# Log sums in quarters of the array, and a scan that delivers scaled states, in a kernel of decayed linear attention and two feed-forward layers

## The chip, the cores and the metric

The kernel runs on 1 core of one Trainium2 chip. The metric is the device time of one execution in microseconds (us). TensorE is PE in the rows (PEld is its weight load), VectorE is DVE, ScalarE is ACT, GpSimd is POOL, SyncE is SP.

## The reference

Three stages follow each other. `B, H, S, D` are 4, 8, 768, 48; the slots are 32 (8 experts of 4), the hidden widths 1024 and 2048.

```python
def _attn_ref(r, k, v, w, u):
    for t in range(S):
        kt, vt, rt, wt = (k[:, :, t], v[:, :, t], r[:, :, t], w[:, :, t])
        cur = np.einsum('bhd,bhe->bhde', u[None] * kt, vt)
        y[:, :, t] = np.einsum('bhd,bhde->bhe', rt, state + cur)
        state = wt[:, :, :, None] * state + np.einsum('bhd,bhe->bhde', kt, vt)

def _moe_ref(x, phi, w1, w2):
    logits = x @ phi
    d = softmax of logits over the tokens
    slot_input = d.T @ x
    slot_out[e] = np.maximum(slot_input[e] @ w1[e], 0.0) @ w2[e]
    c = softmax of logits over the slots
    return c @ slot_out

def _moe2_ref(x, w_in, w_out):
    h = x @ w_in
    g = h * (1.0 / (1.0 + np.exp(-1.702 * h)))
    return g @ w_out
```

All arrays are float32. The two softmax lines are shortened here.

## The kernel before, in words

Each engine has its own program, written out in order, and they meet at semaphores. The attention works on 16 steps, each a pair of heads of one batch (`pair`). A pair's two heads lie at partitions 0 to 47 and 64 to 111 (`HOFF` is 64, `DP` 112). The 768 tokens are 6 chunks (`NC`) of 128 (`P`).

The decays of a chunk are turned into products of powers. ScalarE takes the logarithm of w (`logs`, L473), TensorE adds it up along the tokens by a product with the constant `tri` (`log_sums`, L897), with the middle token of the chunk (`MID`, 64) as origin: column t of `tri` sums the logs from t to the middle with a minus, or from the middle to t with a plus, and column 64 is zero. ScalarE takes exp of both signs (`exps`, L498 and L500) into `pinv` and `pw`, 129 columns a chunk. VectorE multiplies k by `pinv` and r by `pw` (`front`, L701 and L703) and works out `fdec`, the decay from one chunk's middle to the next's (L705).

Inside a pair TensorE goes in this order: transposes of k (L977), in three of four pairs transposes of the batch before's x (L917), transposes of the previous pair's y (L956), the updates of the state by each chunk (L992, into `bank5`, laid out e outside and chunk inside), the scores k times r (L1010), the log sums of the next pair (L897), the states into y (L1033) and the values into y (L1041). Every f32 product shows as two passes in the trace.

Between the updates and the states into y, ScalarE spreads `fdec` over `frep` (`spread_decay`, L515), VectorE runs one scan over all chunks (L712: state = frep * state + update, 240 elements, the zero in the first chunk's column starts each row anew), and ScalarE scales each chunk's state by `fdec` in five copies into `sc` (`scaled_states`, L523), whose semaphore `scaled` TensorE waits for before the states into y. VectorE then adds the bonus part to the previous pair's y (`x_out`, L749 and L751), masks the scores (L718) and does the next pair's `front`, then the bonus sums (L735, L738). GpSimd multiplies for the bonus (L446, L450).

In the pairs with `xg == G3`, two of them in the PE's loop over batches before the last one, the slots' logits of the previous batch (`slot_logits`, L936) go to the upper half of `bank5` after the scores, ScalarE copies them (`lgt_evacuate`, L545), and TensorE transposes them (`token_logits`).

SP's queue fetches ahead with two buffers each: r and k (`load_rk`, L321) when the states into y of two pairs before are done, v and k by tokens (`load_vk`, L327) when that pair's values and bonus are done, w and r by tokens (`load_wr`, L332) when its x is out, with the first layer's weights (L336, L341) in between. After the attention come the slots, the experts (L1131, L1151), and from about 180 us on the second feed-forward layer (L1202, L1231, L1235), which this change leaves alone.

## Time and profile before

| | us |
|---|---|
| median of 3 runs | 400.38 (399.33 to 401.03) |
| profiled execution, its time | 400.66 |
| its span from the first to the last instruction | 398.9 |
| TensorE busy | 390.8 (98%) |
| VectorE busy | 242.9 (61%) |
| ScalarE busy | 187.7 (47%) |
| GpSimd busy | 49.0 (12%) |

The busy times are unions over the whole span; they say little of a stage. The attention runs to about 136 us, the slots and experts to about 176, the last layer to the end. DMA moves 68.66 MB, nearly all of it before 176 us. The granted TensorE clock is 0.999 on average.

### The profile page before, as it was taken

Reading aid. Unit: us, or ns where it says so; the run is one execution under the profiler, and the core shown is the slowest. Engines: PE = TensorE matmul, PEld = TensorE weight load, DVE = VectorE, ACT = ScalarE, POOL = GpSimd, SP = SyncE. Lnnn points to the kernel's source line nnn. Section 1 sums busy time; section 2 is a strip of 40 time slices with the busy share of each in tenths; the row PEclk is TensorE's granted clock in tenths of the full one; section 3 lists DMA queues with packets and bytes.
Section 4 is the critical chain, followed back from the end, with each engine's and each line's share of the span. In section 5 each row is a group of like instructions: output and inputs, shape, how many; then the busy total and the mean of one; then the engine's idle time right before and its main releaser. Section 6 shows DMA issues by size and latency. Waiting matters only on the chain.

```text
span 398.9 us, 8722 instructions
## 1 busy us (share of the span) xinstructions
PE 390.8 (98%) x3290; PEld 312.0 (78%) x3290; DVE 242.9 (61%) x453; ACT 187.7 (47%) x418; POOL 49.0 (12%) x50
## 2 busy tenths in 40 slices
PE   7998999999999999999999999999999999999996
PEld 6887888888888743458888888888888888888885
DVE  4888886978788765257765454454545545455451
ACT  4787887878787523065443222422332242223221
POOL 3532442235223200000000000000000000000000
PEclk9999999999999999999999999999999999999999
DMA  8999999999999899930000100200020020002002
GB/s 288 391 359 395 371 362 364 321 354 392 326 364 362 352 424 398 411 163 2 1 2 31 48 2 0 80 0 1 0 79 0 0 79 2 0 2 79 0 2 79
DMA packets 15859, 68.66 MB, mean 172 GB/s; under 512 B 1744, under 2 KB 2896, under 8 KB 14800
## 3 DMA queue, kind: packets, MB, share of 16 engines
q1 hardware_dynamic: 15824, 68.18, 44.5%
q8 instruction: 24, 0.39, 0.4%
q14 instruction: 11, 0.09, 0.1%
HBM read 63.46 MB, written 4.72 MB: 171 GB/s over the span
## 4 chain that ended last, share of the span: by engine, by line
PE 94%; DMA 2%; DVE 1%; issue 1%; ACT 1%; POOL 0%; ACTq 0%; DVEq 0%; SPq 0%; POOLq 0%
PE bank L1231 32%; PE bank L1235 16%; PE bank L1010 6%; PE bank L897 6%; PE bank L1202 6%; PE bank L1041 5%; PE bank L1033 3%; PE bank L1131 3%; PE bank L1151 3%; PE bank L992 2%; PE bank L977 2%; DMA nat<-nat_in 2%; PE bank L956 1%; PE bank L917 1%; PE bank L936 1%; PE bank L894 1%
## 5 line engine op out<-in xcount | busy, mean ns | idle before, releaser
L628 ACT ACTIVATE ring<-bank 128x512 f32<-128x512 f32 x96 | 57.3, 598 | 138.4 <-PE bank L1202 138.3
L866 DVE CAST g_split<-ring 128x512 fp32r<-128x512 f32 x96 | 41.0, 427 | 88.2 <-ACT ring L628 88.2
L1231 PE MATMUL bank<-g_split,wo_hi 128*128 128x512 f32 x285 | 80.1, 389 | 0.0
L1231 PE MATMUL bank<-g_split,wo_lo 128*128 128x512 f32 x285 | 80.0, 389 | 0.0
L1235 PE MATMUL bank<-g_split,wo_hi 128*128 128x512 f32 x285 | 80.0, 389 | 0.0
L868 DVE TENSOR_TENSOR g_split<-ring,g_split 128x512 fp32r<-128x512 f32 x96 | 66.5, 693 | 3.3
L1231 PEld LDWEIGHTS bank<-g_split,wo_lo 128*128 128x128 f32 x285 | 53.5, 188 | 11.1
L1235 PEld LDWEIGHTS bank<-g_split,wo_hi 128*128 128x128 f32 x285 | 53.5, 188 | 11.1
L1231 PEld LDWEIGHTS bank<-g_split,wo_hi 128*128 128x128 f32 x285 | 53.4, 188 | 11.2 <-DVE g_split L866 0.2
L1202 PE MATMUL bank<-cst,mst 128*128 (+1 forms) x96 | 37.4, 391 | 0.0
L446 POOL TENSOR_TENSOR nat<-nat 128x576 f32<-128x576 f32 x16 | 22.6, 1412 | 79.9 <-DMA nat<-nat_in 33.9
L718 DVE TENSOR_TENSOR at<-bank,causal 128x512 f32<-128x512 f32 x48 | 30.0, 681 | 1.5 <-PE bank L1010 1.5
L523 ACT ACTIVATE sc<-tsum,fdec 112x48 f32<-112x48 f32 x80 | 23.5, 369 | 5.1 <-DVE tsum L712 5.1
L1010 PE MATMUL bank<-rk 48*128 48x128 f32 x384 | 25.7, 280 | 0.0
L897 PE MATMUL bank<-tri,lw 128*112 128x129 f32 x192 | 25.7, 284 | 0.0
L897 PEld LDWEIGHTS bank<-tri,lw 128*112 128x112 f32 x192 | 22.4, 180 | 2.6 <-issue 1.1
L1041 PE MATMUL bank<-at,nat 128*48 128x128 f32 x384 | 24.3, 276 | 0.0
L1010 PEld LDWEIGHTS bank<-rk 48*128 48x128 f32 x384 | 22.7, 187 | 1.2 <-issue 0.4
L450 POOL TENSOR_TENSOR nat<-nat,ub 128x576 f32<-128x576 f32 x16 | 22.5, 1409 | 1.3
L1041 PEld LDWEIGHTS bank<-at,nat 128*48 128x48 f32 x384 | 20.2, 123 | 3.0 <-issue 3.0
L701 DVE TENSOR_TENSOR rk<-rk,pinv 112x768 f32<-112x768 f32 x15 | 14.4, 959 | 13.0 <-ACT pinv L498 12.8
L1202 PEld LDWEIGHTS bank<-cst,mst 128*128 128x128 f32 x96 | 17.9, 188 | 3.9 <-ACT mst L623 0.3
(162 smaller groups left out, 424.9 us busy)
## 6 DMA issues: line engine op xcount, KB each, us to landing
nat<-nat_in SPq DMA_DIRECT2D x32, 576.0 KB, 6.5
rk<-rk_in SPq DMA_DIRECT2D x16, 768.0 KB, 6.5
ring<-w_in SPq DMA_DIRECT2D x16, 768.0 KB, 8.1
w2a<-w_in SPq DMA_DIRECT2D x4, 1536.0 KB, 7.4
out_t<-ring SPq DMA_DIRECT2D x5, 768.0 KB, 3.5
ring<-w_in SPq DMA_DIRECT2D x6, 512.0 KB, 6.8
ring<-win_in SPq DMA_DIRECT2D x3, 1024.0 KB, 7.8
ring<-wout_in SPq DMA_DIRECT2D x4, 768.0 KB, 13.4
```

The source lines that it names most:

```text
L446: g.tensor_tensor(rb, rb, kb, ALU.mult).then_inc(bonus_done, 1)
L523: ins = a.activation(sc[0:DP, c, :], tsum[0:DP, :].rearrange("p (e c) -> p e c", e=D)[:, :, c], ACT.Copy, scale=fdec[0:DP, c:c + 1])
L628: a.activation(gact[:, s % NG, :], bank[6 + s % 2][:, :], ACT.Gelu_apprx_sigmoid).then_inc(g_done, 1)
L718: v.tensor_tensor(at[:, 4 * q:4 * q + 4, :], bank[2 + q][:, :].rearrange("p (u t) -> p u t", u=4), causal[:, :].unsqueeze(1).to_broadcast( ...
L866: v.tensor_copy(g_hi[:, s % NG, :], gact[:, s % NG, :]).then_inc(ghi_done, 1)
L868: v.tensor_tensor(g_lo[:, s % NG, :], gact[:, s % NG, :], g_hi[:, s % NG, :].bitcast(F32), ALU.subtract).then_inc(glo_done, 1)
L897: return t.matmul(bank[c // G3][0:DP, (c % G3) * (P + 1):(c % G3 + 1) * (P + 1)], lw[:, c, 0:DP], tri[:, :], start=True, stop=True)
L1010: ins = t.matmul(bank[2 + u // 4][:, P * (u % 4):P * (u % 4 + 1)], k[rows, P * c:P * (c + 1)], r[rows, P * c:P * (c + 1)], start=True, sto ...
L1041: ins = t.matmul(bank[6 + q][half:half + D, P * (c // 2):P * (c // 2 + 1)], nat[s.slot][:, 0, HD * c + D * h:HD * c + D * (h + 1)], at[:, ...
L1202: t.matmul(bank[6 + s % 2][:, :], mst[:, P * f:P * (f + 1)], cst[:, bass.ds((2 * it + n) * TB, TB)], start=True, stop=True).then_inc(h_don ...
L1231: t.matmul(bank[3 * par + o][:, :], wo[:, f, P * o:P * (o + 1)], g_hi[:, s % NG, :], start=(f == 0 and wo is wo_hi), stop=False)
L1235: ins = t.matmul(bank[3 * par + o][:, :], wo_hi[:, f, P * o:P * (o + 1)], g_lo[:, s % NG, :], start=False, stop=(f == FC - 1))
```

## The change

The log sums of a chunk become four products of 64 rows, 64 or 48 channels and 64 columns: the rows and columns before and after the middle token, each head apart. The column of the middle token is no longer computed; it is set to one in `pinv` and `pw` at the start. The sums of the earlier half of all chunks lie in one bank and those of the later half in another, and the exponentials read them bank by bank. The scan covers 6 columns of each row (288 elements): it adds the update to the state and multiplies by the next decay, the sixth column being zero, and its output is `sc` itself, which TensorE reads with a step of 6 elements. The copies of `scaled_states` and the semaphore `scaled` are gone; their waits are on `state_done`, `inter_done` and `frep_done`. The slots' logits inside the loop move to the last 128 columns of banks 6 and 7, which hold y: they wait for x of the previous pair, and the states into y wait for their copy. Warm-up products go to another bank.

```diff
-        tsum = sb(gen1, "tsum", [P, D * (NC - 1)])
-        frep = sb(gen1, "frep", [P, D * (NC - 1)])
-        sc = sb(gen1, "sc", [P, NC - 1, D])
+        sc = sb(gen1, "sc", [P, D, NC])
+        frep = sb(gen1, "frep", [P, D, NC])
...
+            src = [bank[half][0:DP, 0:NC * MID].rearrange("p (c t) -> p c t", c=NC) for half in range(2)]
+            tokens = [slice((MID + 1) * half, (MID + 1) * half + MID) for half in range(2)]
...
+                    for half in range(2):
+                        ins = a.activation(pinv[0:DP, chunks, tokens[half]], sums2[half], ACT.Exp, scale=-1.0)
...
-                    a.activation(pinv[0:DP, G3 * q:G3 * (q + 1), :], src[q], ACT.Exp, scale=-1.0).then_inc(inv_done, 1)
+                    a.activation(pinv[0:DP, :, tokens[q]], src[q], ACT.Exp, scale=-1.0).then_inc(inv_done, 1)
...
-            def scaled_states(s):
-                act.wait_ge(state_done, s.i + 1)
...
-                for c in range(NC - 1):
-                    ins = a.activation(sc[0:DP, c, :], tsum[0:DP, :].rearrange("p (e c) -> p e c", e=D)[:, :, c], ACT.Copy, scale=fdec[0:DP, c:c + 1])
-                ins.then_inc(scaled, 1)
...
+            def lgt_evacuate_beside_y(b):
+                act.wait_ge(lgt_done, b + 2)
+                act.wait_ge(logit_done, b + 1)
+                for j in range(2):
+                    ins = a.activation(lgT[0:G3 * NS, P * j:P * (j + 1)], bank[6 + j][0:G3 * NS, BANK - P:BANK], ACT.Copy)
+                ins.then_inc(lgt_out, 1)
...
+            v.memset(pinv[:, :, MID:MID + 1], 1.0).then_inc(mid_set, 1)
+            v.memset(pw[:, :, MID:MID + 1], 1.0).then_inc(mid_set, 1)
...
-                    dve.wait_ge(scaled, s.i)
-                v.tensor_tensor_scan(tsum[0:DP, :], frep[0:DP, :], bank[5][0:DP, 0:D * (NC - 1)], 0.0,
-                                     ALU.mult, ALU.add).then_inc(state_done, 1)
+                    dve.wait_ge(inter_done, s.i)
+                v.tensor_tensor_scan(sc[0:DP, :, :].rearrange("p e c -> p (e c)"), bank[5][0:DP, 0:D * NC],
+                                     frep[0:DP, :, :].rearrange("p e c -> p (e c)"), 0.0, ALU.add, ALU.mult).then_inc(state_done, 1)
...
-            def log_sum(c):
-                return t.matmul(bank[c // G3][0:DP, (c % G3) * (P + 1):(c % G3 + 1) * (P + 1)], lw[:, c, 0:DP], tri[:, :],
-                                start=True, stop=True)
+            def log_sum(c, banks, col):
+                for half in range(2):
+                    rows = slice(MID * half, MID * (half + 1))
+                    for h in range(HP):
+                        ch = slice(HOFF * h, HOFF if h == 0 else DP)
+                        ins = t.matmul(bank[banks[half]][ch, MID * col:MID * (col + 1)], lw[rows, c, ch],
+                                       tri[rows, (MID + 1) * half:(MID + 1) * half + MID], start=True, stop=True)
+                return ins
...
+            def slot_logits_beside_y():
+                for m in range(CM):
+                    for j in range(2):
+                        for g in range(G3):
+                            ins = t.matmul(bank[6 + j][NS * g:NS * (g + 1), BANK - P:BANK], phi[:, m, :], xT[:, m, 2 * g + j, :],
+                                           start=(m == 0), stop=(m == CM - 1))
+                ins.then_inc(lgt_done, 1)
...
-                    pe.wait_ge(state_done, s.i + 1)
-                    slot_logits(bank[5][:, LOGIT:LOGIT + 2 * P])
+                    pe.wait_ge(x_done, 2 * s.i)
+                    slot_logits_beside_y()
...
+                if xg == G3 and n1 is not None:
+                    pe.wait_ge(lgt_out, b + 1)
...
-                pe.wait_ge(scaled, s.i + 1)
+                pe.wait_ge(state_done, s.i + 1)
...
-                        ins = t.matmul(bank[6 + c % 2][half:half + D, P * (c // 2):P * (c // 2 + 1)], sc[rows, c - 1, :],
+                        ins = t.matmul(bank[6 + c % 2][half:half + D, P * (c // 2):P * (c // 2 + 1)], sc[rows, :, c - 1],
```

How the instructions stand on TensorE from the updates of the first pair to the values, before:

```order
L992 MATMUL bank<-nat,kcn 48x48 x10
L1010 MATMUL bank<-rk 128x128 x12
L897 MATMUL bank<-tri,lw 112x129 x6
L1033 MATMUL bank<-rk,sc 48x128 x10
L1041 MATMUL bank<-at,nat 48x128 x12
```

and after, the end of the log sums of one pair and what follows them (the last 4 of 24 log sums; a bank's number stands behind its name):

```order
L907 MATMUL bank0<-tri,lw 64x64
L907 MATMUL bank0<-tri,lw 48x64
L907 MATMUL bank1<-tri,lw 64x64
L907 MATMUL bank1<-tri,lw 48x64
L1054 MATMUL bank7<-rk0,sc 48x128 x2
L1054 MATMUL bank6<-rk0,sc 48x128 x2
L1062 MATMUL bank6<-at,nat0 48x128 x6
L1062 MATMUL bank7<-at,nat0 48x128 x6
```

Six products of 112 channels became 24 in fours of alternating width, two to each bank; nothing else changed places.

On ScalarE, the second pair, before:

```order
L506 ACTIVATE kcn<-bank 128x448
L508 ACTIVATE kcn<-bank 128x112
L515 ACTIVATE frep<-fdec 112x4x48
L473 ACTIVATE lw<-nat 128x12x48
L523 ACTIVATE sc<-tsum,fdec 112x48 x5
L498 ACTIVATE pinv<-bank 112x387 x2
L500 ACTIVATE pw<-bank 112x387 x2
L570 ACTIVATE yts<-bank 112x384 x2
```

and after:

```order
L511 ACTIVATE kcn<-bank 128x448
L513 ACTIVATE kcn<-bank 128x112
L520 ACTIVATE frep<-fdec 112x5x48
L472 ACTIVATE lw<-nat 128x12x48
L503 ACTIVATE pinv<-bank 112x6x64 x2
L505 ACTIVATE pw<-bank 112x6x64 x2
L573 ACTIVATE yts<-bank 112x384 x2
```

The five scalings between the logarithm and the exponentials are gone; the rest keeps its order.

## Rows read from the trace of the kernel before

**Rows 1.** Busy time (instructions) by engine in four stretches, granted clock, DMA share, rate.

```profile
core 0: us, PE busy (x) PEld busy (x) DVE busy (x) ACT busy (x) POOL busy (x), PEclk, DMA share, GB/s
8.00:40.00 32.00, 30.07 (x476) 26.34 (x475) 25.66 (x46) 24.20 (x64) 11.27 (x8) 1.00 0.99 382
40.00:128.00 88.00, 86.94 (x1310) 76.08 (x1309) 72.70 (x128) 70.63 (x185) 31.05 (x22) 1.00 0.96 359
128.00:136.00 8.00, 8.00 (x122) 6.45 (x117) 5.97 (x13) 4.39 (x12) 2.82 (x2) 1.00 0.83 309
136.00:168.00 32.00, 31.84 (x324) 13.07 (x326) 16.07 (x33) 8.06 (x16) 0.00 (x0) 1.00 1.01 413
```

**Rows 2.** Chain of waits, start and length in us: first scores, one period, last scores.

```profile
9.83 1.54 PE bank L1010 x24
...
80.28 1.54 PE bank L1010 x24
81.81 1.50 PE bank L897 x12
83.32 0.79 PE bank L1033 x20
84.11 1.45 PE bank L1041 x24
85.56 0.63 PE bank L977 x5
86.18 0.66 PE bank L917 x6
86.84 0.58 PE bank L956 x6
87.42 0.22 issue
87.64 0.66 PE bank L992 x20
88.29 1.54 PE bank L1010 x24
...
129.72 1.54 PE bank L1010 x24
```

**Rows 3.** Waits: engine, line, waited for; us in total, times, longest.

```profile
ACT pinv L498 <- PE bank L897: 9.1, 14, 1.1
ACT lw L473 <- DMA nat<-nat_in: 7.5, 9, 2.0
```

**Rows 4.** L1033 alone (states into y), its first two slices of time.

```profile
core 0: us, PE busy (x) PEld busy (x), PEclk, DMA share, GB/s
83.24:83.28 0.04, 0.03 (x4) 0.03 (x4) 1.00 0.73 307
83.28:83.39 0.11, 0.11 (x4) 0.11 (x8) 1.00 1.09 447
```

**Rows 5.** Groups by line: shapes, count | busy us, mean ns | idle before.

```profile
L523 ACT ACTIVATE sc<-tsum,fdec 112x48 f32<-112x48 f32 x80 | 23.5, 369 | 5.1 <-DVE tsum L712 5.1
L498 ACT ACTIVATE pinv<-bank 112x387 f32<-112x387 f32 x30 | 13.1, 490 | 9.3 <-PE bank L897 9.1
L712 DVE TENSOR_TENSOR_SCAN tsum<-frep,bank 112x240 f32<-112x240 f32 x16 | 10.4, 652 | 6.8 <-PE bank L992 4.8 <-ACT frep L515 2.1
L1033 PEld LDWEIGHTS bank<-rk,sc 48*48 48x48 f32 x320 | 9.7, 119 | 2.4 <-issue 0.6
L515 ACT ACTIVATE frep<-fdec 112x192 f32<-112x192 f32 x16 | 9.1, 569 | 0.0
L545 ACT ACTIVATE lgT<-bank 96x256 f32<-96x256 f32 x4 | 1.5, 372 | 0.7 <-PE bank L936 0.7
```

**Rows 6.** Timeline around the first slots' logits: start, length, what.

```profile
64.59 0.45 DVE L751 TENSOR_TENSOR x_all<-bank,nat 128x288 f32 x1
64.85 1.46 ACT L523 ACTIVATE sc<-tsum,fdec 112x48 f32<-112x48 f32 x5
...
65.05 1.50 PE L936 MATMUL bank<-xT,phi 128*32 128x256 f32 x18
```

More of the change, by code:

```diff
@@ L160, in decay_attention_soft_moe_gelu_kernel @@
         const_dve = sem("const_dve")
+        mid_set = sem("mid_set")
         first_ln = sem("first_ln")
@@ L474, in logs @@
                              w.rearrange("p (c e) -> p c e", e=D), ACT.Ln).then_inc(ln_done, 1)
-            src = [bank[q][0:DP, 0:G3 * (P + 1)].rearrange("p (c t) -> p c t", c=G3) for q in range(2)]
+            src = [bank[half][0:DP, 0:NC * MID].rearrange("p (c t) -> p c t", c=NC) for half in range(2)]
+            tokens = [slice((MID + 1) * half, (MID + 1) * half + MID) for half in range(2)]
             def first_logs():
@@ L490, in first_exps @@
                     act.wait_ge(logsum_done if q else first_logsums, 1)
-                    a.activation(pinv[0:DP, chunks, :], src[q], ACT.Exp, scale=-1.0).then_inc(inv_done, 1)
-                    a.activation(pw[0:DP, chunks, :], src[q], ACT.Exp).then_inc(exp_done, 1)
+                    sums2 = [bank[2 * q + half][0:DP, 0:G3 * MID].rearrange("p (c t) -> p c t", c=G3) for half in range(2)]
+                    for half in range(2):
+                        ins = a.activation(pinv[0:DP, chunks, tokens[half]], sums2[half], ACT.Exp, scale=-1.0)
+                    ins.then_inc(inv_done, 1)
+                    for half in range(2):
+                        ins = a.activation(pw[0:DP, chunks, tokens[half]], sums2[half], ACT.Exp)
+                    ins.then_inc(exp_done, 1)
             def exps(s):
@@ L514, in spread_decay @@
                     act.wait_ge(state_done, s.i)
-                a.activation(frep[0:DP, :].rearrange("p (e c) -> p c e", e=D)[:, 1:NC - 1, :],
-                             fdec[0:DP, 0:NC - 2].unsqueeze(2).to_broadcast([DP, NC - 2, D]), ACT.Copy).then_inc(frep_done, 1)
-            def scaled_states(s):
-                act.wait_ge(state_done, s.i + 1)
-                if not s.first:
-                    act.wait_ge(inter_done, s.i)
-                for c in range(NC - 1):
-                    ins = a.activation(sc[0:DP, c, :], tsum[0:DP, :].rearrange("p (e c) -> p e c", e=D)[:, :, c], ACT.Copy, scale=fdec[0:DP, c:c + 1])
-                ins.then_inc(scaled, 1)
+                a.activation(frep[0:DP, :, :].rearrange("p e c -> p c e")[:, 0:NC - 1, :],
+                             fdec[0:DP, :].unsqueeze(2).to_broadcast([DP, NC - 1, D]), ACT.Copy).then_inc(frep_done, 1)
             def xt_evacuate(b, c):
@@ L560, in pair @@
                 elif xg == G3:
[L561 removed]
+                    lgt_evacuate_beside_y(b)
                 if s.after(1) is not None:
@@ L670, in _ @@
             v.memset(own[:, :, :], 0.0).then_inc(const_dve, 1)
-            v.memset(frep[:, :], 0.0).then_inc(const_dve, 1)
+            v.memset(frep[:, :, :], 0.0).then_inc(const_dve, 1)
+            v.memset(pinv[:, :, MID:MID + 1], 1.0).then_inc(mid_set, 1)
+            v.memset(pw[:, :, MID:MID + 1], 1.0).then_inc(mid_set, 1)
             v.memset(strip[:, :], 0.0).then_inc(const_dve, 1)
@@ L683, in first_front @@
             def first_front():
+                dve.wait_ge(mid_set, 2)
                 dve.wait_ge(ld_rk[0], 16)
@@ L894, in stay_warm @@
                     t.matmul(bank[to][:, 0:2 * P], ones_b[:, 0:P], ones_b[:, :], start=True, stop=True)
-            def log_sum(c):
-                return t.matmul(bank[c // G3][0:DP, (c % G3) * (P + 1):(c % G3 + 1) * (P + 1)], lw[:, c, 0:DP], tri[:, :],
-                                start=True, stop=True)
+            def log_sum(c, banks, col):
+                for half in range(2):
+                    rows = slice(MID * half, MID * (half + 1))
[4 more added lines that the diff above has]
+                return ins
             def first_log_sums():
@@ L911, in log_sums @@
                 for c in range(NC):
-                    ins = log_sum(c)
+                    ins = log_sum(c, (0, 1), c)
                 ins.then_inc(logsum_done, 1)
@@ L1049, in _ @@
             pe.wait_ge(const_pool, 1)
-            stay_warm(15, 1)
+            stay_warm(15, 4)
             pe.wait_ge(const_pool, 5)
             first_log_sums()
-            stay_warm(3, 3)
+            stay_warm(3, 4)
             pe.wait_ge(const_dve, 4)
```

13 lines of the change are left out of this document (5 added, 8 removed).

## The prediction

> **What bounds the kernel now.** I read the stretches first. From 8 to 128 us all sixteen head pairs run, in periods of one pair [rows 1]: TensorE is busy 30.07 of 32.00 and 86.94 of 88.00 us, at a granted clock of 1.00. The same rows hold a second thing: the DMA share is 0.99 and 0.96, with 382 and 359 GB/s. After the attention, from 136 to 168 us, the share is 1.01 at 413 GB/s, so 1.01 is what "always busy" looks like in this column. Vector work fills 72.70 of 88 us, ScalarE 70.63. So TensorE is first, the DMA engines stand some 2 to 5% behind it, and nothing else is near.
>
> Then the chain of waits [rows 2]. The scores of the first pair start at 9.83 us and those of the last at 129.72, fifteen periods of 7.99 us on average. The chain goes through TensorE alone in the usual period: scores 1.54, log sums 1.50, states into y 0.79, values 1.45, then transposes 0.63, 0.66, 0.58, then updates 0.66, from 80.28 to 88.29 us. It has one gap, 0.22 us, in front of the updates. No ScalarE row is in it: the five scalings of the states are hidden.
>
> Last the waits of the other engines [rows 3]. ScalarE waits for the log sums 14 times, 9.1 us in all, and before its logarithm 9 times for a load of `nat`, 7.5 us in all, at most 2.0. This last row matters most: in 9 of 15 pairs the decay of the next pair arrives just as it is wanted. The loads are fetched one buffer turn ahead and are as late as a buffer turn allows.
>
> **The change part by part.**
>
> *Log sums.* Before, each of 6 chunks is a product of 128 rows by 112 channels by 129 columns. It shows as 12 passes (two for each f32 product) one behind the other. After, there are 24 products, 48 passes, each in one of four quarters of the array, 64 columns long. How long is a round of passes in different quarters? The states into y use the same quarters: 20 passes, of which the busiest quarter has 6, in 0.79 us; the updates do 20 passes in two column halves, 10 rounds of 48 columns, in 0.66; the values 12 rounds of 128 in 1.45 [rows 2]. That four quarters do start together is seen in the first 0.04 us of the states into y, which hold four starts, with no further one in the next 0.11 [rows 4]. Two unknowns, columns and a fixed cost S at each change of the array's shape, fit these rows: at 0.83 ns a column (two clocks at 2.4 GHz, granted 1.00) the values take 1.28 + S, the updates 0.40 + S, the states 0.64 + S and the old log sums 12 x 129 x 0.83 ns = 1.28 + S, so S is 0.15 to 0.26 us, mostly near 0.17. The new log sums are 12 rounds of 64: 0.64 + 0.17 = 0.81. The states into y behind them have the same quarter shape, so their own S mostly goes: 0.79 becomes about 0.65. Together 2.29 becomes 1.46, **0.83 us less TensorE time for each pair**. Over 15 periods 12.4 us.
>
> *Scaling.* The five ScalarE copies go: 5 x 369 ns, in the chain of none. They free ScalarE, but cost nothing today [rows 5]. They would be late once the log sums are short: in the stretch shown they end at 66.31 us, 1.26 us after the scores do (65.05) [rows 6], and the new log sums end 0.81 after. So removing them is what lets the first gain through. No term of its own.
>
> *Scan.* 288 elements in place of 240, with sum and product in the other order. 652 ns [rows 5] times 288/240 is 782: +0.13 at most, 0 at least. I take +0.10. The zero column of `frep` restarts each row of states. The decay spread grows from 192 to 240 elements, 569 ns: 0 to +0.14, I take +0.10. Both lie beside TensorE's path: VectorE is busy 72.70 us in eleven periods, 6.6 us each [rows 1], 6.7 with the longer scan, and ScalarE 6.4 less the 1.5 of the scalings. Below a period of 7.2 us that is cover enough. Cost nothing; VectorE would be next if the periods went under 7 us, since its scan, x and masks stand between the updates and the next k.
>
> *Strided states.* The states are now read as weights with a step of 6 elements. No row shows a weight load with a step. The nearest is the same load without one, 119 ns [rows 5]. The bound from below is 0. From above, a doubled load would make a round 240 in place of 109 ns, six rounds, +0.8 us a pair. I take 0: the element count is the same, and the row it is nearest to is the unstrided one. The upper end stays for the range.
>
> *Exponentials.* Same elements in 4 instructions; the first pair has 8 in place of 4, at 192 elements each. Between half of 490 ns and the whole [rows 5] that is 0 to +2 us on ScalarE in the first pair. Partly covered by shorter log sums: +0.2.
>
> *Slots' logits.* In the two batches in the loop these are now 36 passes of 128 columns in place of 18 of 256: the same columns. They wait for x of the pair before. That ended at 65.04 us where they began at 65.05 [rows 6]; with the slower scan and spread they wait 0.2 us, twice. Behind them TensorE waits for the copy of the logits, today 372 ns [rows 5], then two smaller ones; the log sums in between (0.81) cover that. +0.4 in all, on TensorE alone. The last pair keeps its own place for them.
>
> *The DMA.* Nothing is added or removed on SP's queue; each load is merely asked for earlier. All loads of the attention need their time: 382 x 32 + 359 x 88 = 43.8 MB. By TensorE alone the periods would be 7.99 - 0.83 = 7.16 us, and 2.9 MB a pair at that pace is 408 GB/s, more than either stretch shows. So **the DMA engines end the gain**. What they can give is their idle time: (1.01 - 0.99) x 32 + (1.01 - 0.96) x 88 = 5.0 us, if packets keep the pace they have. If the pace rises to that of the first stretch (382/0.99 x 1.01 = 390 GB/s), 43.8 MB need 112.3 in place of 120 us, 7.7 us less.
>
> *After the attention* nothing changes. Its loads begin when the attention's buffers come free, so they move with it; between 128 and 136 us the share is 0.83 [rows 1], so that a backlog of 1 us has room.
>
> **Sum.** 400.66 us of the profiled execution, less 5.0, plus 0.2 for the start (the 0.4 of the logits lies where DMA binds): 395.9. The median of the runs is 0.28 lower, so 395.6; I say **395.5 us**.
>
> **Rivals.**
>
> *TensorE keeps the bound.* The packets go faster when asked for earlier, as after 136 us (413 GB/s). For it: the first stretch had 382. Against: 96% share already. -12.4 + 0.2 + 0.4, so 388.6. Chance 0.18.
>
> *A floor under the starts.* The Trainium skill, TensorE: Matmul & The Clock Gate, section "Wait — 56ns, not 53.3ns?", says that start-to-start of matmuls never falls below about 25 ns; by that page 48 passes are 1.2 us and the block would save 0.3 us a pair, an estimate. Against this rule the trace has four starts within 0.04 us [rows 4]. By rows alone the same case is this: 48 passes at the 33 ns of the updates (0.66/20) are 1.58, the block 2.23 in place of 2.29, nothing but 0.06 x 15 = 0.9 us: 399.6. Chance 0.05.
>
> *No gain.* A load arrives one latency after its buffer is free, whatever TensorE does, and a doubled weight load would eat the rest (0.83 - 0.8). For it: the 9 waits for `nat`. Against: rk and the first weights are asked for after the states into y, which now come 0.8 us earlier. 399 to 401. Chance 0.13.
>
> *Slower.* The four quarters do not run together, because here the halves of a chunk have 64 and 48 channels and two row halves, where the states' have 48 everywhere. Then 48 passes of 53 ns one behind the other are 2.56 us, the block 2.56 + 0.17 + 0.65 = 3.4 in place of 2.29, and 15 x 1.1 = 16 us: 417. It decides from 34 ns a pass on. Chance 0.12.
>
> **Numbers.** DMA-bound forecast 0.52, its own range 392.5 to 398. Below 398.4 (0.5% below the median, about what a measurement of this kernel can tell from no change) lie the forecast, the TensorE case and 0.03 of the floor and no-gain cases, 0.73; within 0.5% the rest of these two, 0.15; above, 0.12. The range leaves out the slower case and the best end of the TensorE case: 389 to 400.
>
> **What would show it.** Right: the log sums' group in the chain near 0.8 us and the states near 0.65; the DMA share of 40 to 128 us at 1.00 or more; TensorE with gaps before the updates or log sums where it had none; waits for `nat` longer. Scan near 750 ns. Wrong: log sums above 1.4 us, or weight loads of the states well over 120 ns (slower or no gain); or a DMA rate over 395 GB/s with periods of 7.2 us (TensorE bound).

## The result, and the profile after

| | before | after |
|---|---|---|
| median, us | 400.7 (4 runs) | 408.78 (4 runs, 408.15 to 414.3) |
| ratio, 95% interval | | 1.0203 (1.0168 to 1.0237) |
| profiled execution, us | 400.66 | 408.57 |
| span, us | 398.9 | 406.8 |
| TensorE instructions in the page (matmul passes) | 3290 | 3902 |

The change makes the kernel about 2% slower. The forecast was 395.5 us, 1.2% faster. The execution of 414.3 us was a slow one, and the ratio leaves it out.

First the stretches of the changed kernel, the columns as in [rows 1]:

```profile
core 0: us, PE busy (x) PEld busy (x) DVE busy (x) ACT busy (x) POOL busy (x), PEclk, DMA share, GB/s
8.00:40.00 32.00, 26.42 (x590) 23.00 (x588) 24.92 (x43) 17.83 (x43) 11.31 (x8) 1.00 0.93 358
40.00:128.00 88.00, 78.77 (x1700) 70.06 (x1701) 71.39 (x123) 52.13 (x124) 31.03 (x22) 0.98 0.93 351
128.00:136.00 8.00, 6.07 (x73) 5.21 (x66) 4.09 (x7) 4.65 (x11) 1.49 (x2) 0.79 0.66 259
```

TensorE was busy 98.8% of 40 to 128 us before and is busy 89.5% now. The DMA share fell too, from 0.99 and 0.96 to 0.93 and 0.93, where the forecast wanted 1.00. So neither TensorE nor the DMA engines, which were to end the gain, are busy all the time. Something else stops both.

The chain of waits says where. Three places of it, start and length in us; L1029 are the scores, L907 the log sums, L1054 the states into y, L1062 the values, L996, L928 and L975 the transposes, L1011 the updates. The chain can show fewer instructions of a group than there are (45 of 48 log sums):

```profile
9.38 1.54 PE bank L1029 x24
...
26.18 0.85 PE bank L907 x45
27.03 0.25 PE bank L1054 x8
27.28 2.76 issue
30.05 0.68 PE bank L1054 x12
...
49.25 1.54 PE bank L1029 x24
50.79 0.85 PE bank L907 x45
51.64 0.69 PE bank L1054 x20
...
56.38 1.54 PE bank L1029 x24
...
93.28 0.57 PE bank L1062 x7
93.84 1.93 issue
95.78 1.14 PE bank L1062 x17
96.92 0.94 PE bank L996 x5
97.87 1.28 PE bank L928 x6
...
137.55 1.54 PE bank L1029 x24
```

The period from 49.25 to 56.38 is what the forecast described: log sums 0.85, states 0.69, values 1.45, 7.13 us in all. The like period of before, from 47.73 to 55.45, took 7.72; the 7.99 of the forecast is a mean that holds the slots' logits and some waits as well.

```profile
47.73 1.54 PE bank L1010 x24
...
55.45 1.54 PE bank L1010 x24
```

But others have a hole in the middle of a group: TensorE has done 8 of 20 states into y, stops for 2.76 us, and does the other 12, though nothing was waited for between them in the program. "issue" is the profile's word for time in which an engine waits for nothing that the profile shows. There are seven such holes over 1 us up to 137.55: 1.65 at 20.00, 2.76 at 27.28, 1.72 at 60.69, 1.45 at 69.09, 1.93 at 93.84, 1.06 at 121.42 and 1.93 at 128.22, 12.5 us in all. Before there was none of that length; the one "issue" of its period, 0.22, stands between two groups [rows 2].

From the first scores to the last it is 137.55 - 9.38 = 128.2 us now and 129.72 - 9.83 = 119.9 before. Fifteen clean periods of 7.13 would be 107.0. The 21.2 us between are the 12.5 of the holes; some 3.2 of a lower clock behind two of them (96.92 to 101.00 and 130.62 to 134.96: transposes of 0.94, 1.28 and, L975, 1.12 where [rows 2] has 0.63, 0.66 and 0.58; the granted clock of 128 to 136 us is 0.79, a mix of the levels 2.4 and 1.2 GHz, after TensorE had stood for 1.93 us); and 5.5 that have little to do with the holes. Of these, 4.2 come with the three groups of slots' logits (67.04, 102.69 and 136.12), which before has too; 1.2 are the two pairs behind the first two of these groups (7.74 us each, where the chain runs from 71.17 to 79.01 through ScalarE's exponentials and VectorE's work); 1.1 is a wait for one load of nat (6.86 us at 35.81); and the first four periods, which have no transposes of x, are 1.2 shorter than 7.13. Without the holes and the lower clock the stretch would be 112.5 us, 7.4 less than before. From the last scores to the end nothing changed: 269.2 us before, 269.3 after.

The waits after, in the form of [rows 3], and the groups that answer to [rows 5]:

```profile
PEld bank L1054 <- issue: 5.2, 3, 2.9
ACT pinv L503 <- PE bank L907: 24.9, 15, 2.4
ACT lw L472 <- DMA nat<-nat_in: 4.5, 6, 2.2
```

```profile
L718 DVE TENSOR_TENSOR_SCAN sc<-bank,frep 112x288 f32<-112x288 f32 x16 | 12.1, 756 | 18.8 <-PE bank L1011 13.9 <-ACT frep L520 4.8
L1054 PEld LDWEIGHTS bank<-rk,sc 48*48 48x48 f32 x320 | 11.7, 163 | 5.7 <-issue 5.2 <-DVE x_all L757 0.5
L520 ACT ACTIVATE frep<-fdec 112x240 f32<-112x240 f32 x16 | 10.4, 649 | 0.0
```

ScalarE and VectorE wait longer for TensorE (24.9 us for log sums in place of 9.1), and the logarithm waits less for its load (4.5 in place of 7.5). TensorE is late, not the data.

**What the holes have in common.** From one to the next it is 252 passes and weight loads, or a multiple of that. Two stretches between the beginnings of neighbouring holes (a third, 121.30 to 128.10, has 129 passes and 126 loads):

```profile
19.90:27.20 7.30, 5.59 (x127) 4.87 (x126) 5.64 (x10) 3.24 (x9) 2.64 (x2) 1.00 1.01 407
60.60:69.00 8.40, 6.47 (x128) 5.63 (x126) 5.75 (x11) 3.71 (x10) 2.83 (x2) 1.00 1.00 390
```

126 weight loads in each, and the passes to them (those that lie across an edge of the window are counted too): 252. The trace also keeps the semaphore instructions on TensorE's queue, four between two such holes. With all records of TensorE counted from the first, the seven holes stand before number 704, 960, 2240, 2496, 3520, 4544 and 4800: whole multiples of 256 apart, every one. The page has a queue that brings instructions:

```profile
q8 instruction: 28, 0.46, 0.4%
```

28 packets, 0.46 MB, that is 16 KB each; before there were 24 and 0.39 MB. (A second such queue, q14, has 10 packets here and 11 before, so it doesn't follow TensorE's count.) An instruction thus takes 64 bytes if a packet holds 256 of them. The change has 612 more passes, each with a weight load, 1224 instructions more; four packets more hold 1024. And the packets stand where the holes end: of the three windows 21.7 to 27.3, 27.3 to 28.6 and 28.6 to 30.0 us the middle one alone has one of q8, as its queues show, and TensorE resumes at 30.05, 1.4 us behind that window's end.

```profile
q1 hardware_dynamic: 120, 0.41, 91.7%
q8 instruction: 1, 0.02, 5.2%
q14 instruction: 1, 0.01, 1.6%
```

The single packets of q8 in the trace say more. Take the places of the attention that are 256 instructions apart, whether TensorE stops there or not. In the change exactly one packet lies between each two neighbouring ones. It begins 1.1 to 5.8 us after the first of the two places and takes some 1.0 us. (In the kernel before it is 0.6 to 4.3 us, and once 1.2 us ahead of the place.) In all seven holes TensorE goes on 1.3 to 1.5 us after the packet's end, and at no place, in any kernel of this study, does it go on sooner than 1.2 us after it. Before, the shortest such time is 3.2 us: each packet is there in good time.

So **theory A**: TensorE's instructions arrive in blocks of 256 over the same 16 DMA engines as the data; a block is asked for only when the one before the last is used up, it waits its turn behind the loads of r, k, nat and weights, and it lands several us later (from the beginning of the hole at 20.00 to the end of the next at 30.05 pass 10.1 us, and 256 instructions). A usual pair of before has 238 instructions in the trace (117 passes, as many weight loads and 4 semaphore instructions) and one of the change has 310 (48 log-sum passes in place of 12). At 7.72 us a pair a block lasts 8.3 us, at 7.13 us only 5.9. (The expectations below count 264 and 336, and the other kernels likewise 26 too many a pair. The differences between kernels are right; their times for a block are too short and their counts per us too high. The numbers outside of the expectations are those of the trace.) **The rival B**: the quarter-shaped products themselves cost, by a change of the array's shape or by their weight loads.

The Trainium skill, Runtime: NRT & Kernel Launch, section Instruction fetch mechanics, says that the instruction memory is refilled in blocks of 16 KiB, 256 instructions, over a DMA queue of the engine's own, and that crossing a block's end is "mostly hidden". The 16 KB packets and the 256 instructions between the holes agree with the block; the holes of 1 to 2.8 us speak against "hidden".

### The profile page after: what moved, and what is told of

The parts are those of the page before. It is cut to its first block, busy times and chain, and to the rows that moved or that the text cites. A ratio compares the mean times of both kernels' runs of the same rounds, so it can differ in the third digit from the quotient of the medians.

```text
span 406.8 us, 9860 instructions
## 1 busy us (share of the span) xinstructions
PE 384.6 (95%) x3902; PEld 307.0 (75%) x3902; DVE 245.4 (60%) x455; ACT 166.3 (41%) x344; POOL 49.1 (12%) x50
## 4 chain that ended last, share of the span: by engine, by line
PE 87%; issue 5%; DVE 4%; ACT 2%; DMA 2%; DVEq 0%; POOL 0%; ACTq 0%; SPq 0%; POOLq 0%
PE bank L1252 32%; PE bank L1256 16%; PE bank L1223 5%; PE bank L1062 5%; PE bank L1029 4%; PE bank L907 3%; PE bank L1152 3%; PE bank L1172 3%; PE bank L996 2%; PE bank L1054 2%; PE bank L1011 2%; DMA nat<-nat_in 2%; PE bank L975 2%; PE bank L928 2%; PE bank L900 1%
## 5 line engine op out<-in xcount | busy, mean ns | idle before, releaser
L1062 PE MATMUL bank<-at,nat 128*48 128x128 f32 x384 | 26.1, 281 | 7.0 <-issue 6.4
L1062 PEld LDWEIGHTS bank<-at,nat 128*48 128x48 f32 x384 | 21.1, 125 | 10.2 <-issue 7.1
L1029 PE MATMUL bank<-rk 48*128 48x128 f32 x384 | 25.7, 280 | 0.0
L1029 PEld LDWEIGHTS bank<-rk 48*128 48x128 f32 x384 | 22.7, 187 | 1.2 <-issue 0.4
L718 DVE TENSOR_TENSOR_SCAN sc<-bank,frep 112x288 f32<-112x288 f32 x16 | 12.1, 756 | 18.8 <-PE bank L1011 13.9
L503 ACT ACTIVATE pinv<-bank 112x384 f32<-112x384 f32 x30 | 13.1, 491 | 24.9 <-PE bank L907 24.9
L573 ACT ACTIVATE yts<-bank 112x384 f32<-112x384 f32 x32 | 15.8, 494 | 16.2 <-PE bank L1062 15.4
L707 DVE TENSOR_TENSOR rk<-rk,pinv 112x768 f32<-112x768 f32 x15 | 15.4, 1024 | 7.0 <-ACT pinv L503 6.5
```

Of the source, the lines that this page charges most:

```text
L573: a.activation(yts[0:DP, cols], bank[6 + q][0:DP, 0:cols.stop - cols.start], ACT.Copy).then_inc(yt_out, 1)
L1029: ins = t.matmul(bank[2 + u // 4][:, P * (u % 4):P * (u % 4 + 1)], k[rows, P * c:P * (c + 1)], r[rows, P * c:P * (c + 1)], start=True, sto ...
L1062: ins = t.matmul(bank[6 + q][half:half + D, P * (c // 2):P * (c // 2 + 1)], nat[s.slot][:, 0, HD * c + D * h:HD * c + D * (h + 1)], at[:, ...
```

## The experiments

The median of the kernel before was 400.3 to 401.5 us in the sets of runs; every ratio is to that of the same set.

**x1: the change, with the log sums undone.** Scan, states, scaling and slots' logits stay as changed.

```diff
-                for half in range(2):
-                    for h in range(HP):
-                        ins = t.matmul(bank[banks[half]][ch, ...], lw[rows, c, ch], tri[rows, ...], start=True, stop=True)
+                return t.matmul(bank[c // G3][0:DP, (c % G3) * (P + 1):(c % G3 + 1) * (P + 1)], lw[:, c, 0:DP], tri[:, :],
+                                start=True, stop=True)
```

> The change with its log sums put back to six products of 128 rows and 129 columns. Theory A (TensorE's instruction blocks of 256 come too late, because the quarters raise the instructions of a pair from 264 to 336): the mid-group pauses of 1.3 to 2.9 us go, 24 or 25 instruction packets, time 399 to 402. Rival B (the pauses come from the scan's strided output read as weights, or from the logits' new place): the pauses stay, 406 or more.

Measured: 400.87 us, ratio 1.0003 (0.9983 to 1.0023), 24 instruction packets, no hole in a group.

**x2: before, with the quarter log sums alone.** The products are those of the change.

> The kernel before with the log sums in quarters and nothing else of the change. Theory A: pauses like those of the change, 27 or 28 instruction packets, time 405 to 411. Rival B: no pauses, the log sums' gain is seen in part, 393 to 398.

Measured: 407.61 us, ratio 1.0175 (1.0131 to 1.0219), 28 instruction packets. Its chain of waits behind the log sums that begin at 26.23 us (L1048 states into y):

```profile
27.09 0.44 PE bank L1048 x8
27.53 2.62 issue
30.15 0.66 PE bank L1048 x12
```

The same hole behind the same eight passes of the states as in the change, although scan, scaling and states are those of before. Its holes over 0.7 us are five, 9.4 us in all. So the quarter log sums make the loss, all of it as far as the intervals tell; the other parts of the change are worth nothing by themselves that could be measured (x1: at most 0.2% either way). This doesn't yet tell A from B.

**x3 and x9: row halves.** Log sums as 12 products of 64 rows and all 112 channels: 262 instructions per pair.

```diff
-                    for h in range(HP):
-                        ch = slice(HOFF * h, HOFF if h == 0 else DP)
-                        ins = t.matmul(bank[banks[half]][ch, ...], lw[rows, c, ch], ...
+                    ins = t.matmul(bank[banks[half]][0:DP, MID * col:MID * (col + 1)], lw[rows, c, 0:DP], ...
```

> The change with the log sums split in two row halves only (12 products of 64 rows, 112 channels, 64 columns): 48 instructions where the quarters have 96. Theory A: a block lasts 6.5 us or more, few pauses or short ones; the log sums take 1.1 to 1.3 us a pair; 396 to 402. Rival C (row halves into two banks are the trouble, however many instructions): as slow as the change, 407 or more.

> The kernel of x3 once more, in more rounds: log sums as 12 products of 64 rows and all 112 channels, so a pair issues 288 instructions in place of 336 and a block of 256 lasts some 6.4 us. Its profile had log sums of 1.14 to 1.31 us, no pause in the middle of a group, and three waits of 5.7 to 6.7 us for a load of nat: the DMA bound of the forecast. Theory A: 398 to 400.5 us, ratio 0.993 to 0.999, the small gain that the DMA engines allow. Theory B (quarters as such cost) says nothing else here. A ratio of 1.000 or more would say that the DMA bound takes all.

Measured: x3 400.46 us, ratio 0.9967 (0.9929 to 1.0006); x9 400.61 us, 0.9981 (0.9952 to 1.0011), both 25 packets and no hole in a group. The chain of x9 (L905 log sums, L1027 scores):

```profile
11.28 1.54 PE bank L1027 x24
12.81 1.14 PE bank L905 x24
...
25.56 7.25 DMA nat<-nat_in
```

Two row halves overlap in part: 24 passes in 1.14 us, 48 ns each, where the prediction's 0.83 ns a column gives 53 for 64 columns one behind the other; the 12 passes of twice the rows and columns took 1.50. And this is what the kernel looks like where the loads end the gain: the first period is 6.86 us, but a load of nat asked for at 25.56 lands 7.25 us later, and the stretches 8 to 40 and 40 to 128 have a DMA share of 0.97 and 0.98. Log sums that are 0.36 us shorter would give 5.4 us in fifteen periods; from the first scores to the last (11.28 to 129.16) it is 2.0 us less than before, and of the whole time 0 to 0.5%.

**x4 and x5: padding.** The kernel before with some 70 more instructions per pair that do nothing: no-operations in x4, increments of a semaphore nobody waits for in x5.

> The kernel before with 70 no-operation instructions a pair on TensorE's queue, two behind each score, value and log sum product and one behind each product of the states into y; no arithmetic is changed. Theory A: a block lasts about 6.2 us in place of 7.8, pauses of 1 to 3 us in the middle of groups where before had none, 28 instruction packets in place of 24, 404 to 412. Rival B: no pauses, 400 to 402. If a no-operation itself costs time in TensorE's queue, the groups are longer throughout, without pauses in their middle.

> The kernel before with some 70 semaphore increments per pair added on TensorE's queue, on a semaphore that nobody waits for, spread over log sums, scores and values; no matmul is changed, so a pair issues some 336 instructions in place of 264. Theory A (instructions arrive in blocks of 256, the next block is fetched only once the one before is crossed into, and the fetch waits its turn behind the data): pauses of 1.3 to 2.9 us at the block boundaries although the matmuls are those of before, 405 to 410 us, ratio 1.012 to 1.022, and 28 or so instruction packets in place of 24. Theory B (what costs is the quarter-shaped matmuls themselves, their array shape or their weight loads): 400.5 to 402 us. If the increments leave the compiled program, the packets stay at 24 and nothing is told.

x4: 401.48 us, 1.0019 (0.9987 to 1.005), with the 24 packets of before: the no-operations were not in the program that ran, so it tells nothing. x5: 484.81 us, 1.209. The increments are no free padding. Its scores (L1016) with their 24 increments, two behind each of 12 products:

```profile
87.22 3.52 PE bank L1016 x24
```

3.52 us in place of 1.54, so some 82 ns for an increment. A pair takes up to 13.4 us with that and a block about 11, the DMA share of 40 to 128 us is 0.62, and there are no holes: both theories allow it, and my number was wrong.

**x6: shorter transfers.** The change, each load of the attention given as two of 64 partitions.

```diff
+                for z in range(2):
+                    sp.dma_start(rk[slot][64 * z:64 * (z + 1), :, :], rk_in[bass.ds(n, 1), 64 * z:64 * (z + 1)]...
```

> The changed kernel with each load of rk, v/k, w/r and of the first expert weights given as two transfers of 64 partitions; same bytes, smaller packets per row of the queue. Theory A: the fetch of the next instruction block waits behind the packets that are already on the DMA engines; if the wait is set by the size of what lies ahead of it, the pauses get shorter, 399 to 406 us; if it is set by the bytes alone, 407 to 410. Theory B: 408 to 409, no change, as TensorE's instructions are the same.

Measured: 468.88 us, 1.1711 (1.1653 to 1.1769).

```profile
40.00:128.00 88.00, 66.90 (x1185) 59.04 (x1183) 48.71 (x84) 36.95 (x85) 21.52 (x16) 0.79 1.02 236
```

The DMA engines are always busy (1.02) at 236 GB/s, where [rows 1] has 413 at 1.01. A transfer into 64 partitions moves at little over half the rate, so the kernel waits for its loads above all, and its time tells nothing of A. Its holes do. The longest in the middle of groups:

```profile
26.03 3.90 issue
...
102.43 3.95 issue
...
184.15 4.67 issue
```

They stand before the same instructions as in the change (704, 2496 and 4800), and a packet of q8 begins up to 12.3 us after the place before it, where the change had 5.8 at most. Yet TensorE asks for only some 28 instructions per us here, fewer than in the kernel before. So slow data transfers make the blocks late even at a low pace: the pace of the instructions counts, and so does what the DMA engines carry beside them. The Trainium skill, SBUF — State Buffer, section "Door 1: The DMA port swizzle (why `[64,N]` ≈ `[32,N]`)", says that partitions 0 to 63 are reached through 8 of the 16 ports; the rate of 236 GB/s, 57% of 413, agrees with it.

**x7 and x8: the DMA engines given room.** The loads of w1 go (16 of 768 KB, 12.6 of the attention's 43.8 MB, so 29% and not the 40 of the expectation), and GpSimd fills the buffer with zeros; in the changed kernel (x7) and in the one before (x8).

```diff
-                sp.dma_start(ring[:, bass.ds(m, 1), half], w1_in...).then_inc(ld_w1, 16)
+                g.memset(ring[:, n // 2, (n % 2) * (CM * FE // 2):(n % 2 + 1) * (CM * FE // 2)], 0.0).then_inc(ld_w1, 1)
```

> The changed kernel without the loads of the first expert weights (w1) during the attention: GpSimd fills that buffer with zeros instead, so the first layer of the experts computes with zeros. That takes some 40 percent of the attention's DMA traffic away. Theory A with the engines as the forecast had them: fetches land in time, no pauses in the middle of groups, periods near 7.2 us, and this kernel is 8 to 13 us faster than the one before with the same cut (x8). Theory B: pauses stay, it is slower than x8.

> The kernel before without the loads of the first expert weights, buffer filled with zeros by GpSimd; the first layer of the experts computes with zeros. Both theories: TensorE bound as before, periods 7.95 to 8.0 us, 395 to 401 us. It is the partner of x7: the difference x7 minus x8 is what the change is worth when the DMA engines have room, minus 8 to minus 13 us by theory A, above 0 by theory B.

Measured: x7 394.17 us, 0.9815 (0.9776 to 0.9854); x8 399.41 us, 0.9959 (0.9940 to 0.9978). With room on the DMA engines the same change is 5.2 us faster (394.17 - 399.41), not 8 slower. So the quarter products don't cost by themselves, and B falls in its plain form. The holes are shorter and fewer, but there, and at the same numbers as in the change. The chain of x7 (L1063 values):

```profile
55.05 1.23 PE bank L1063 x20
56.28 0.82 issue
57.10 0.43 PE bank L1063 x4
```

Its others are 1.18 at 63.79 and 0.90 at 117.85. The gain is under the 8 to 13 that I wrote. The holes take 2.9 us of it, and one load of nat, 6.63 us from 31.79 in the chain, came late even here: the DMA share of the first stretch is still 0.87.

**x10: quarters for three chunks, row halves for three.** 286 instructions per pair.

```diff
-                    for h in range(HP):
-                        ch = slice(HOFF * h, HOFF if h == 0 else DP)
+                    for h in range(HP) if c % 2 else range(1):
+                        ch = slice(HOFF * h, HOFF if h == 0 else DP) if c % 2 else slice(0, DP)
```

> The changed kernel with quarters for three of the six chunks and row halves for the other three: 312 instructions per pair, same results, same columns. Theory A (blocks of 256 instructions against a fetch of 5 to 8 us): a block lasts some 5.9 us, so some of the boundaries pause, shorter and fewer than with 336: 401 to 406 us, between x3 (400.5) and the change (408.8). Theory B (each quarter-shaped product costs): 404 to 405, half way, but with slower log sums in place of pauses.

Measured: 406.34 us, 1.0130 (1.0089 to 1.0170), 27 packets. Just above the 401 to 406 of A and the 405 of B, and for two reasons at once (L907 log sums, L1062 values):

```profile
44.21 1.23 PE bank L1062 x18
45.44 1.16 issue
...
51.18 1.64 PE bank L907 x30
```

The mix of shapes runs in 1.64 us, longer than the six full products (1.50) and than either shape alone (0.85, 1.14), of which half and half would be 1.0. So products of different shapes in turn lose what each shape gains; whether they don't run side by side or each change of shape costs, this run doesn't tell. That is 16 x 0.14 = 2.2 us over x1. The holes (1.16, 1.07 and 0.71) are 2.9. Together 400.9 + 5.1 = 406.0.

**x11 and x12: 1.5 MB less in the attention.** The early loads of the last expert's second weights go behind the fifth expert's; with row halves (x11) and with the change's quarters (x12).

```diff
-                    if q == 1:
-                        load_w2_early(m - 1)
...
             sp.dma_start(w2_fifth[:, :], w2_in[G4]).then_inc(ld_w2[G4], 16)
+            sp.dma_start(w2_early[:, :], w2_in[NE - 1]).then_inc(ld_w2[NE - 1], 16)
```

> The kernel of x9 with the early loads of the last expert's second weights (8 x 192 KB, 1.5 MB) taken out of the attention and given in one load behind the fifth expert's. The DMA bound of the forecast says: the attention moves 3.4 percent less, so up to 3.4 percent of its 120 us, 4 us, come back if the DMA engines bind: 395 to 398.5 us. If the load is late where it is used, the gain is given back there: 399 to 402 us. If the DMA engines don't bind, as x9.

> The changed kernel (quarters, 336 instructions per pair) with the same move of 1.5 MB out of the attention. Theory A: the fetch of instructions still waits behind data, pauses stay at the boundaries, slightly shorter: 404 to 408 us. If data volume decides and not the fetch (theory C: the pauses are late loads under another name), it would gain as x11 does and come under 401 us.

Measured: x11 400.64 us, ratio 0.9959 (0.9933 to 0.9986); x12 407.19 us, 1.0114 (1.0054 to 1.0174). x12 has holes like the change (six over 1 us, 3.04 at 27.39 the longest), so it isn't the volume of data alone. The profile of x11 is of a slower execution (403.63 us). It has one short stop at a block's place, 0.53 us at 111.97, and two of "issue", 1.28 and 0.98, that are not at such a place but between two groups, transposes and updates; what these waited for stays open. x11 is the one full kernel of this study that beats both, by 0.4%; its interval overlaps that of x9, so what the moved load adds isn't shown.

**x13 and x14: more instructions, no quarters.** The kernel before, every product of scores and values split into two of 64 columns, 334 instructions per pair; x14 is the same without w1.

```diff
-                    ins = t.matmul(bank[2 + u // 4][:, P * (u % 4):P * (u % 4 + 1)],
-                                   k[rows, P * c:P * (c + 1)], r[rows, P * c:P * (c + 1)], start=True, stop=True)
+                    for z in range(0, P, 64):
+                        ins = t.matmul(bank[2 + u // 4][:, P * (u % 4) + z:P * (u % 4) + z + 64],
+                                       k[rows, P * c:P * (c + 1)], r[rows, P * c + z:P * c + z + 64], start=True, stop=True)
```

> The kernel before, log sums and all else untouched, with each product of the scores and of the values split into two of 64 columns: same columns, same shapes of the array, 360 instructions per pair in place of 264. Theory A (blocks of 256 instructions, fetched behind the data): a block lasts some 5.7 us, and pauses of 1 to 3 us begin in the middle of groups, each a block of 256 instructions after a crossing; 405 to 415 us over and above what the two groups themselves grow by (to be read from their rows, times 16). Theory B (what costs is the quarter shape of the log sums): no pauses; 400.5 us plus the growth of the two groups.

> The kernel of x13 without the loads of the first expert weights, as in x8 (buffer filled with zeros by GpSimd, so the experts' first layer computes with zeros). Theory A: the fetches land sooner, so x14 minus x8 is smaller than x13 minus the kernel before, by most of x13's pauses. Theory B: the two differences are the same within 1.5 us.

Measured: x13 423.35 us, 1.0550 (1.0492 to 1.0609); x14 421.91 us, 1.0526 (1.0473 to 1.0579). The difference of the two differences (22.5 over x8, 23.1 over before) is nothing, as B says. But the chain shows why no verdict follows (L1011 scores, L1043 values):

```profile
65.52 2.87 PE bank L1011 x48
...
70.69 1.56 PE bank L1043 x48
...
74.69 2.87 PE bank L1011 x48
```

The scores grew from 1.54 to 2.87 us: 60 ns a pass of 64 columns, where one of 128 took 64; each has a weight load of 128 columns. With the values' 0.11 that is 16 x 1.44 = 23.0 us, all that x13 lost. The period is 9.17 us, so a block lasts 7.0, and the DMA share of 40 to 128 us fell to 0.85. TensorE asked for fewer instructions per us than the change does, 36 in place of 43, and there are no holes; no packet came later than 3.6 us after the place before it. What counts under A is instructions per us. That was the test to make.

**x15: the count and the pace of the change, without its shape.** Row halves (x9), with the values alone split into 64 columns: 310 instructions per pair.

> The kernel of x9 (row halves, 288 instructions per pair, 400.6 us, no pauses) with each product of the values split into two of 64 columns: 336 instructions per pair, as many as in the change, with no quarter-shaped log sum. In x13 the same split took the values from 1.45 to 1.56 us, so the split itself costs 16 x 0.11 = 1.8 us. x13 also showed that the count per pair is not the measure but the count per microsecond: 39 per us there, without pauses; 47 per us in the change. Here 336 in some 7.5 us, 45 per us. Theory A: pauses of 1 to 3 us in the middle of groups, 256 instructions after the crossing before; 405 to 411 us. Theory B (the quarter shape costs): no pauses, 400.6 + 1.8 = 402.4 us, at most 403.5.

Measured: 404.6 us, ratio 1.0117 (1.0068 to 1.0166), 28 packets. The chain (L1061 values):

```profile
28.73 1.29 PE bank L1061 x36
30.02 0.91 issue
30.93 0.61 PE bank L1061 x12
...
36.96 0.58 PE bank L1061 x15
37.54 1.25 issue
38.79 1.16 PE bank L1061 x33
```

and between the two holes:

```profile
30.10:37.60 7.50, 6.55 (x126) 5.92 (x126) 5.86 (x11) 3.77 (x10) 2.82 (x2) 1.00 1.02 410
```

Holes in the middle of a group, 256 instructions apart, without one quarter-shaped log sum. Their sum with a third (0.81 at 128.00) is 3.0 us, and 402.4 + 3.0 is 405.4; measured 404.6. A fourth of 0.67 at 45.15 would make it 406.1, so the holes don't add up in full. All four stand at a block's place, a multiple of 256 from the numbers above. B's bound of 403.5 lies below the run and also below its fastest execution, 404.14. A's lower end of 405 was 0.4 too high: at 41 per us the holes are shorter than at 43.

The kernels together, a period being that of a usual pair without a hole, the share that of the DMA engines from 40 to 128 us, and the holes those over 0.7 us at a block's place in the chain of the attention:

| kernel | instructions per pair | period, us | per us | DMA share | holes | ratio |
|---|---|---|---|---|---|---|
| x6, the change, split loads | 310 | some 11 | 28 | 1.02 at 236 GB/s | 8, to 4.7 us | 1.171 |
| before | 238 | 7.72 | 31 | 0.96 | none | 1 |
| x1, full sums | 238 | 7.77 | 31 | 0.96 | none | 1.000 |
| x9, row halves | 262 | 7.6 | 34 | 0.98 | none | 0.998 |
| x11, row halves, late w2 | 262 | 7.5 | 35 | 0.93 | none | 0.996 |
| x13, split scores and values | 334 | 9.17 | 36 | 0.85 | none | 1.055 |
| x10, mixed | 286 | 7.76 | 37 | 0.93 | 3, to 1.2 us | 1.013 |
| x2, quarters alone | 310 | 7.8 | 40 | 0.92 | 5, to 2.6 us | 1.018 |
| x15, row halves, split values | 310 | 7.6 | 41 | 0.95 | 3, to 1.3 us | 1.012 |
| x12, the change, late w2 | 310 | 7.6 | 41 | 0.93 | 6, to 3.0 us | 1.011 |
| the change | 310 | 7.13 | 43 | 0.93 | 7, to 2.8 us | 1.020 |
| x7, the change without w1 | 310 | 7.0 | 44 | 0.77 | 3, to 1.2 us | 0.982 |

Holes come with the pace of instructions and with the load on the DMA engines, and that is A. What exactly a packet waits for is not seen: with the same share of 0.77 the latest began 3.2 us after its place in x8 and 5.6 in x7. That a block is fetched one block ahead and no earlier is read from the single packets and the places; no run changed the depth. Putting TensorE's pairs in a loop, which might spare the fetches, wasn't tried. The last layer, whose products do run in a loop, hints that it would: from 248 to 345 us q8 has no packet, with TensorE busy throughout.

## Why the prediction was wrong, point by point

*What bounds the kernel now* was read rightly: TensorE first, the DMA engines close behind it. The 7.99 us, though, is a mean with the slots' logits in it; a usual pair took 7.72.

*Log sums and states into y* were right in size. 0.85 and 0.69 us, 1.54 together, where 1.46 was forecast and 2.29 stood before. The quarters run side by side, the rival "slower" by serial quarters fell; its 417 us came from a mechanism that isn't there. 48 passes in 0.85 us also rule out the floor under the starts, at least across quarters: 18 ns each, where the Trainium skill, TensorE: Matmul & The Clock Gate, section "Wait — 56ns, not 53.3ns?", has about 25.

*Scaling* and *Scan*: 756 ns (between 652 and 782), spread 649 (569 + 80), hidden in the usual pair. *Strided states*: the weight load shows 163 ns in place of 119, but the group is 0.69 us and in x1, with the strided states and full sums, nothing is lost: 0 was right. *Exponentials* can't be told from nothing. *Slots' logits*: TensorE waits 0.3 us for x in front of them, where 0.2 was forecast, but the pair behind each of the two groups takes 7.74 us in place of 7.13 (in x7 7.73 and 7.75 in place of 7.0), because there VectorE's work is what the chain goes through. That is 1.2 us that the sum had not; at the longer periods of x1, which has the logits in the same place, nothing of it is seen. *After the attention* nothing changed, as said.

***The DMA* is the step that failed.** It reads "Nothing is added or removed on SP's queue" and goes on as if the data were all that the DMA engines carry. The change adds 72 instructions to a pair on TensorE, the shortened period brings them faster, and TensorE's own instruction blocks come over the same engines. The step costed new passes by what they take on the array, 0.64 + 0.17 us, and never by their number as instructions. The page of before held the line to start from: 24 instruction packets, about one to a period of the attention, beside data at a share of 0.96 to 0.99. The kernels at 34 to 36 instructions per us have no holes and those from 37 on do, so before, at 31, the margin was a fifth of the pace; the change took it up to 43, and that was not looked at. In its place the runs show 12.5 us of holes and 3.2 us at the lower clock behind them, against 7.4 us of periods that are shorter otherwise: 8.3 us slower from the first scores to the last.

The size of the DMA bound itself was off as well. With the holes out of the way (x9) the gain is 0.2% of the time and at most 0.5, where 5.0 us, 1.2%, were forecast from the idle share. The wait of 7.25 us for a load of nat in x9 is what the rival "no gain" described: a load comes a latency after its buffer is free, whatever TensorE does. The idle share of the forecast, 2% and 5% of the two stretches, was not time that a shorter period could have. And the share itself misleads: it is 1.02 at 236 GB/s in x6 and 0.87 at 306 in x7.

## What to carry to other kernels

Where a product is cut into smaller ones that run side by side, count the instructions per us that this asks for, not the columns alone: here all was well up to 36 per us, and from 37 to 44 TensorE stood still for 0.7 to 3 us at three to seven of some twenty blocks of 256. That is no fixed limit: with data transfers at little over half their rate (x6) TensorE stood for up to 4.7 us at 28 per us. Holes in the middle of a group, a multiple of 256 instructions apart, with "issue" as their cause, are the mark of it. "issue" between two groups can be something else, as in x11. Where data keeps the DMA engines over nine tenths busy, prefer the shape with fewer instructions even if its group is longer: row halves, 0.3 us longer and with 48 instructions fewer per pair, lost nothing where quarters lost 2%.

## What the runs showed that I had not expected

- An instruction block of 16 KB waits behind data for its turn. In the seven holes of the change TensorE went on 1.3 to 1.5 us after the packet's end (28.6 to 30.05 in the longest).
- The log sums' 48 passes of 64 columns take 0.85 us, 18 ns each, and products of two shapes in turn lose that: 1.64 us for the mix of x10 against 0.85 and 1.14 for either shape alone.
- A semaphore increment on TensorE costs some 82 ns (x5: 3.52 us for scores of 1.54 with 24 of them).
- Two row halves of 64 rows overlap only in part, 24 passes in 1.14 us.
- Transfers into 64 partitions move 236 GB/s with all DMA engines busy, where those of [rows 1] move 413.
- Behind two stands of 1.93 us TensorE's groups ran up to twice as long for 3 to 4 us (granted clock 0.79 from 128 to 136), so that a hole can cost more than its length; behind the longer one of 2.76 us they didn't (values 1.45 at 30.73).
